# Column sums of attention probabilities: two 64-column groups of 288 columns in PSUM bank 5, in place of four 32-column groups of 144 columns in bank 4

## What is computed

```python
q_pool = q.reshape(B, H, S // factor, factor, D).mean(axis=3)
scores = scale * np.matmul(q_pool, k.transpose(0, 1, 3, 2))
scores = scores - np.max(scores, axis=-1, keepdims=True)
attn = np.exp(scores)
attn = attn / (np.sum(attn, axis=-1, keepdims=True) + 1e-09)
return np.matmul(attn, v).astype(np.float32)
...
x = np.ascontiguousarray(attn_out.transpose(0, 2, 1, 3)).reshape(B * S, H * D)
x = _moe_ref(x=x, **moe_kwargs)
return _moe2_ref(x=x, **moe2_kwargs)
```

## Time and profile before

| | us |
|---|---|
| median of 3 runs | 743.3 |
| the three runs | 743.18 to 743.6 |
| span of the profiled execution, first to last instruction | 738.7 |
| TensorE busy | 724.9 |
| GpSimd busy | 485.1 |
| VectorE busy | 523.4 |
| ScalarE busy | 455.6 |

### The profile page before, as it was taken

How to read it: one execution, slowest core, us unless ns; L and a number is a source line. 1 busy time by engine, 2 the same in 40 slices (tenths; PEclk the granted TensorE clock), 3 DMA queues, 4 the chain that set the end, 5 groups by cost and what they waited for, 6 DMA issues and landing times.

```text
span 738.7 us, 17096 instructions
## 1 busy us (share of the span) xinstructions
PE 724.9 (98%) x6375; PEld 540.5 (73%) x6375; DVE 523.4 (71%) x826; ACT 455.6 (62%) x1008; POOL 485.1 (66%) x431
## 2 busy tenths in 40 slices
PE   7999999999999999999999999999999999999997
PEld 5776777777777777777777677434778888888886
DVE  6888888888888888888888847533894555455542
ACT  3677776776777767767767763214655454545453
POOL 2588888888888888888888873212774444444442
PEclk8999999999999999999999999999999999999999
DMA  5123335334244353353342347899301010101011
GB/s 142 47 59 100 106 95 157 99 111 151 88 120 143 91 155 105 98 164 88 112 151 88 96 140 259 298 387 387 132 1 43 1 43 0 43 0 43 0 43 43
DMA packets 51623, 81.83 MB, mean 111 GB/s; under 512 B 14556, under 2 KB 20572, under 8 KB 51548
## 3 DMA queue, kind: packets, MB, share of 16 engines
q1 hardware_dynamic: 51468, 80.69, 35.0%
q10 hardware_dynamic: 80, 0.13, 0.0%
HBM read 75.94 MB, written 4.79 MB: 109 GB/s over the span
## 4 chain that ended last, share of the span: by engine, by line
PE 93%; DVE 3%; ACT 1%; issue 1%; POOL 1%; DMA 0%; SPq 0%; DVEq 0%; POOLq 0%; ACTq 0%
PE ps L680 20%; PE ps L657 8%; PE ps L987 8%; PE ps L986 8%; PE ps L985 8%; PE ps L625 6%; PE ps L659 5%; PE ps L661 5%; PE ps L663 5%; PE ps L691 3%; PE ps L585 3%; PE ps L975 2%; PE ps L899 2%; PE ps L869 2%; PE ps L590 1%
## 5 line engine op out<-in xcount | busy, mean ns | idle before, releaser
L1072 ACT ACTIVATE probs<-ps 128x576 f32<-128x576 f32 x288 | 183.8, 652 | 44.0 <-PE ps L663 28.9
L1356 DVE TENSOR_REDUCE mx<-ps 128x2 f32<-128x1024 f32 (+1 forms) x160 | 189.2, 1217 | 29.1 <-PE ps L625 27.1
L551 POOL TENSOR_TENSOR g_lo<-g_buf,g_hi 128x384 fp32r<-128x384 f32 x96 | 102.1, 1066 | 100.8 <-ACT g_hi L1245 100.8
L680 PE MATMUL ps<-probs,v_sb 128*64 128x288 f32 x1152 | 146.8, 409 | 0.1
L512 POOL TENSOR_TENSOR p_sum<-p_sum,probs 128x576 f32<-128x576 f32 x93 | 129.1, 1413 | 0.0
L1584 DVE SCALAR_TENSOR_TENSOR v_buf<-u_buf 128x384 f32<-128x384 f32 x96 | 60.2, 627 | 86.7 <-ACT u_buf L1238 86.1
L680 PEld LDWEIGHTS ps<-probs,v_sb 128*64 128x64 f32 x1152 | 79.7, 137 | 56.3 <-issue 5.2
L1238 ACT ACTIVATE u_buf<-ps,half 128x384 f32<-128x384 f32 x96 | 55.8, 582 | 93.7 <-PE ps L975 93.7
L985 PE MATMUL ps<-wo_hi,g_hi 128*128 128x512 f32 x282 | 110.5, 392 | 0.6 <-POOL g_lo L551 0.4
L987 PE MATMUL ps<-wo_lo,g_hi 128*128 128x512 f32 x282 | 110.8, 393 | 0.0
L986 PE MATMUL ps<-wo_hi,g_lo 128*128 128x512 f32 x282 | 110.6, 392 | 0.0
(11 more groups left out here) (214 smaller groups left out, 1251.6 us busy)
## 6 DMA issues: line engine op xcount, KB each, us to landing
pre<-in_moe_w SPq DMA_DIRECT2D x41, 512.0 KB, 4.7
k_raw<-in_k SPq DMA_DIRECT2D x32, 288.0 KB, 3.8
v_sb<-in_v SPq DMA_DIRECT2D x32, 288.0 KB, 2.8
q_raw<-in_q SPq DMA_DIRECT2D x32, 256.0 KB, 3.9
from_x<-in_moe_w SPq DMA_DIRECT2D x9, 512.0 KB, 5.2
p_inv<-inv_dram SPq DMA_DIRECT2D x62, 72.0 KB, 2.6
out<-o_stage SPq DMA_DIRECT2D x34, 128.0 KB, 2.4
staged<-in_moe_w SPq DMA_DIRECT2D x8, 512.0 KB, 5.2
```

The costliest lines, as they stand in the source:

```text
L680: mm = pe.matmul(ps[D * h:D * h + D, 4, 0:HALF], v_sb[n % 2][:, u, :], probs[:, u, HALF * h:HALF * h + HALF], start=(i == 0), stop=(i == N ...
L1072: nc.scalar.activation(dst, ps[:, b0:b0 + 2, 0:HALF], ACT.Exp, scale=SCORE_SCALE).then_inc(exp_done, 1)
L1356: top = nc.vector.tensor_reduce(mx[0:w, NC * t:NC * t + 2], ps[0:w, b:b + 2, :], AX.X, ALU.max)
```

## The change

The branch for all heads but the last does the same as that of the last head: two 64-column groups, 288 queries each, so 2 matmuls for each source where there were 4, each with twice the columns. The result goes to columns 0 to 287 of bank 5 rather than to columns 288 to 431 of bank 4. ScalarE's copy of the sums has 288 columns, not 144; `x_sum` grows and gets another address, and the move to `p_spread` takes 2 rows of 288 numbers, not 4 of 144. The logits of batch 0, which lie in bank 5 too, get a further wait for `x_read` of head 30.

```diff
-    x_sum = at("x_sum", [P, QUAD], 65536)
+    x_sum = at("x_sum", [P, HALF], 73984)
...
-                             x_sum[0:P:SLOTS, :].rearrange("c (p j) -> c p j", j=NT)).then_inc(sums_spread, 16)
+                             x_sum[0:P:D, :].rearrange("c (p j) -> c p j", j=NT)).then_inc(sums_spread, 16)
...
-                        for c in range(4):
-                            mm = pe.matmul(ps[SLOTS * c:SLOTS * c + SLOTS, 4, HALF:HALF + QUAD], ones[:, 0:SLOTS],
-                                           src[:, QUAD * c:QUAD * c + QUAD], start=first, stop=not first)
+                        for h in range(2):
+                            mm = pe.matmul(ps[D * h:D * h + D, 5, 0:HALF], ones[:, :],
+                                           src[:, HALF * h:HALF * h + HALF], start=first, stop=not first)
...
                         pe.wait_ge(phi_loaded, 16)
+                        pe.wait_ge(x_read, HEADS - 1)
                         logits(0, range(0, KD // 2))
...
-                nc.scalar.activation(x_sum[:, :], ps[:, 4, HALF:HALF + QUAD], ACT.Identity,
+                nc.scalar.activation(x_sum[:, :], ps[:, 5, 0:HALF], ACT.Identity,
                                      bias=eps[:, :]).then_inc(x_read, 1)
```

More of the change, by code:

```diff
@@ L66, in soft_moe_chain @@
     KP = (NT - 1) // 2 * P
-    QUAD = SQ // 4
     PIECE = FT * DM // 4
```

## The result

| | median, us | runs | ratio to the kernel before |
|---|---|---|---|
| before | 743.6 | 743.18 to 744.11 (5) | |
| changed | 753.43 | 751.07 to 755.93 (5) | 1.0141, 95% interval 1.0123 to 1.0159 |

The changed kernel is slower by 9.1 to 11.8 us (the interval of the ratio times 743.6). The forecast was 753.5.

A forecast was written before the change was run, and what follows sets the result against it. TensorE was taken to bound the kernel. +0.44 us in the sums and -0.11 at the end of the products with v make 0.33 us a head; 743.3 + 31 x 0.33 = 753.5 us, range 750.7 to 757.2.

The forecast's parts named there:

- TensorE sets the pace and nothing absorbs its time: Attention heads: each 0.1 us added to a head costs 3.1 us; the rival of absorbed time, 743.3 us, had chance 0.04.
- +0.44 us in the sums: Products with ones, each ordinary head: 0.49 + 0.58 us in the new form against 0.27 + 0.36 in the old.
- rival of a smaller drain: Step from the sums to the next job: costs less in ordinary heads than in the last; 750.7 us, chance 0.06.
- streaming alone adds 0.24 us a head: Products with ones: reason given for a chance of only 0.02 that the changed kernel is faster.
- the lower bound: No change of shape costs anything after the sums: 31 x (0.49 - 0.14 - 0.11) = 7.4 us more, 750.7 us.
- -0.11 us at the end of the products with v: First ones weights load 0.24 us ahead of their matmul, without the step from 64 to 32 columns: 0.11 us saved a head.
- Sparing time for the early load: GpSimd's last addition still ends in time for the earlier load of the ones weights, with 0.20 us to spare.
- The 3 late sums of the earlier trace: GpSimd's addition was late 3 times, 1.3 us in all; the saving may be lost there, at most 0.3 us.
- The copy: ScalarE's x_sum copy: 413 ns instead of 375, 0.04 us more, covered by 0.17 us of idle time before the first exponent.
- The side path: Move to p_spread: 4.31 us available, 3.28 needed, so no cost; a late transfer, some 772 us, had chance 0.03.
- The bank, the address, the wait ahead of the logits: Bank 5, x_sum's new address and the wait for x_read of head 30 before the logits: no cost.
- The sum: 31 ordinary heads: 31 x 0.33 = 10.2 us more, added to 743.3 for 753.5 us.

The follow-up runs named there:

- first_twice: Kernel before with the ones product of p_sum done twice (8 more MATMUL records of 144 columns): 750.32 us, ratio 1.0098, stretch 13.75 us.
- ones64_144: Changed kernel with each ones product cut into two of 144 columns, 8 matmuls instead of 4: 752.77 us, ratio to before 1.0144, stretch 13.84 us.
- ones32_288: Changed kernel with ones weights of 32 columns instead of 64, still 288 moving columns: 756.64 us, ratio to before 1.0190, stretch 13.95 us.
- waits_early: Kernel before with the two waits of the ones products moved ahead of the last tile of the products with v: 747.06 us, ratio 1.0060, stretch 13.65 us.
- copy_extra: Changed kernel with an unused third ScalarE copy of 160 columns between the two copies: 756.06 us, ratio to before 1.0181, stretch 13.93 us.
- bank5_only: Kernel before with its four 32-column groups of 144 columns written to bank 5 and copied from there: 742.66 us, ratio 1.0002, stretch 13.48 us.
- copy288_old: Old four groups in bank 5, ScalarE copying 288 columns to x_sum, only 144 used: 741.65 us, ratio to before 0.9994, stretch 13.48 us.

## Why the prediction was right, point by point

- **TensorE sets the pace and nothing absorbs its time**: right. Its waits for exponents stayed as they were (21.5 and 21.8 us), and first_twice shows that 0.26 us more of TensorE's work in a head comes through whole.
- **+0.44 us in the sums**: right. 0.49 + 0.58 against 0.27 + 0.36, and ones64_144 shows that it is the columns. The 0.58 us to line 624 are the last head's, so the rival of a smaller drain is out. One sentence on the chances says that streaming alone adds 0.24 us a head. By the prediction's own rounds it adds 0.98 - 0.49 = 0.49 us; 0.24 is the net of the lower bound.
- **-0.11 us at the end of the products with v**: right (0.10 with more digits, 0.34 to 0.24), and its reason is now tested: ones32_288 brings the gap back, waits_early doesn't remove it. Sparing time for the early load was put at 0.20 us and is about 0.16. The 3 late sums of the earlier trace rows were misread: in the kernel before, the weight path idles the same 0.44 us and the first ones product stands the same 0.34 us behind the last pair in all 31 heads, so these three cost nothing extra. Only head 30 lost something in the changed kernel, where the load starts after the sum and the saving is half gone (0.29 us in place of 0.24). This is the one wait of 0.4 us for line 514.
- **The copy**: right that it is free, wrong in size. I took the record of x_raw, 413 ns, for that of x_sum. But x_raw is a plain copy and x_sum adds a bias, and at 288 columns the two forms take 411 and 495 ns. The rows of before held the answer: its plain copies too take 0.83 ns a column, so x_sum's 375 ns at 144 columns would have become 375 + 144 x 0.83 = 495. Whether the bias or the function makes the 0.08 us was not tested apart. The true size was 0.12 us, not 0.04. The cover is itself 0.12 us larger than the idle time that the rows show, as copy_extra told. The cover held 0.12 us as it would have held 0.04, so the error didn't reach the time; that is luck, in part.
- **The last head** grew by 0.49 us and not by 0.34, which the prediction did not treat apart. From its first scores to the next sums TensorE takes 10.92 us in both kernels, so the longer copy costs nothing there. Counted from the start of head 30's sums, the head gets the 0.44 us of these sums and 0.05 us more, because of the late load (the second source stands 449.34 - 448.81 = 0.53 us behind the first). It doesn't get the saving of 0.10 us, since its own end had the new form already:

```profile
448.80 0.20 PEld L690 LDWEIGHTS ps<-p_sum,ones 128*64 128x64 f32 x4 [0.39 <-POOL p_sum L514]
448.81 0.71 PE L690 MATMUL ps<-p_sum,ones 128*64 128x288 f32 x4
...
449.34 0.66 PE L690 MATMUL ps<-probs,ones 128*64 128x288 f32 x4
```

- **The side path**: right that it costs nothing. The 3.28 us that I took as the transfer's time are no fixed time: in the changed kernel it is 452.96 - 450.95 = 2.01 us at the same place. The number of source rows alone doesn't explain it: first_twice, with four rows, has 2.0 us there, and bank5_only, with four rows too, 3.5. The kernels with two rows have 1.8 to 2.4 us, though, so a part of it may be theirs. Weight pieces go through the same queue there, and I take it that the transfer waits among them; neither was tested.
- **The bank, the address, the wait ahead of the logits**: no cost, as said; bank5_only shows it for the bank and the wait, copy288_old for the address.
- **The sum**: 31 x 0.33 = 10.2 against a measured difference of 9.1 to 11.8. That the median of the five runs, 753.43, stands 0.1 us from the forecast is luck: the runs spread over 4.9 us, and the kernel before has 743.6 over five runs where the forecast stood on 743.3. What bears the forecast is the stretch, 13.83 us as said. The range's upper end, 757.2, stands in none of its sums; the nearest is 756.9. One step in it was not sound: I carried 4.6 us over from span to time. In the profiled execution of the changed kernel there are only 753.43 - 751.5 = 1.9 us. The span of 738.7 came from an execution that was faster than the median, by some 3 us if the 1.9 hold there too. Since I added the difference to the median, the number didn't suffer.

What stays open is why runs of one kernel differ by some us: those of the changed kernel spread over 4.9 us. Those of before spread over 0.9 us beside it, but over 2.9, 3.4 and 1.7 us beside the experiments, so the spread doesn't belong to the change. The clock explains a part in the profiled execution (1.6 us in the slot layer), but the slowest run, 755.93, had a mean clock of 0.998.

## What to carry to other kernels

Where several column groups of TensorE work side by side, count the moving columns that pass one after the other (columns of a record times rounds), and not the matmuls: fewer and larger records with half the groups stream for twice the time (0.98 us a head in place of 0.49 here). Look whether the kernel already runs the new form somewhere, in a last or first iteration, for such rows give the price directly, with the changes of tile shape on both sides. And take the size of a longer operation from rows of the same form (function and bias, not only the shape): here the fixed part differed by 0.08 us between the two forms, while the price of a column was the same.

## What I had not expected of the hardware

- The step from weights of 64 to weights of 32 columns, with 128 rows in both, keeps the next weights from being loaded early and costs 0.10 us (the first ones product 0.34 us behind the last pair in place of 0.24).
- Four MATMUL records of 144 columns in two groups take 0.25 us, four of 288 take 0.49: cutting a matmul in two was worth 0.01 us a head.
- A copy from PSUM on ScalarE costs 0.83 ns for each further column, in both forms (277, 411 and 597 ns at 128, 288 and 512 columns; 375 and 495 ns at 144 and 288 with a bias). It is no shorter on an idle engine than behind another copy (395 and 388 ns at 160 columns), although the next record may start 0.12 us before it ends.
